# Transposes into PSUM, two row buffers, a new order in the MoE steps and 64x64 state products

## The reference

```python
# attention, one state of 64 x 64 per batch and head (4 x 8), 768 tokens each
state = gamma[None, :, None, None] * state + np.einsum('bhd,bhe->bhde', k[:, :, t], v[:, :, t])
y[:, :, t] = scale * np.einsum('bhd,bhde->bhe', q[:, :, t], state)
# MoE on x = y as 3072 tokens x 512, 8 experts, hidden width 1024
e_idx = np.argmax(x @ w_gate, axis=1)
out[mask] = gate_w[mask, None] * eom[mask, e, None] * (np.maximum(x[mask] @ w1[e], 0.0) @ w2[e])
# dense FFN, hidden width 2048
h = x @ w_in
return (h - np.tanh(h)) @ w_out
```

## Time and profile before

| | us |
|---|---|
| median of three runs | 1077.05 |
| lowest, highest | 1075.08, 1082.54 |
| profiled execution, its time | 1083.84 |
| its span, first to last instruction | 1082.1 |
| attention, MoE (from the span's start) | 0 to 145.4, 145.4 to 516 |
| PE, PEld, DVE, ACT, POOL busy in the span | 1037.4, 864.3, 722.2, 312.7, 390.9 |

### The profile page before, as it was taken

How to read it: one execution, slowest core, us unless ns; L and a number is a source line. 1 busy time by engine, 2 the same in 40 slices (tenths; PEclk the granted TensorE clock), 3 DMA queues, 4 the chain that set the end, 5 groups by cost and what they waited for, 6 DMA issues and landing times.

```text
span 1082.1 us, 18080 instructions
## 1 busy us (share of the span) xinstructions
PE 1037.4 (96%) x5424; PEld 864.3 (80%) x5425; DVE 722.2 (67%) x1247; ACT 312.7 (29%) x560; POOL 390.9 (36%) x325
## 2 busy tenths in 40 slices
PE   9999968989999999999789999999999999999998
PEld 8888857878888888787678887888887888888887
DVE  3666674654655556555478768877787886887775
ACT  2222212322323222231123333333334333333333
POOL 4377768585585995935700000000000000000000
PEclk9999988999999999999989999999999999999999
...
GB/s 332 278 315 307 254 152 223 223 240 213 242 234 223 273 262 221 259 204 165 81 10 11 20 39 19 19 0 48 19 10 48 16 13 39 19 0 0 40 1 39
DMA packets 70964, 138.28 MB, mean 128 GB/s; under 512 B 7056, under 2 KB 39184, under 8 KB 70928
## 3 DMA queue, kind: packets, MB, share of 16 engines
...
...
## 4 chain that ended last, share of the span: by engine, by line
PE 80%; DVE 8%; DMA 6%; issue 2%; ACTq 1%; ACT 1%; POOL 0%; DVEq 0%; SPq 0%; POOLq 0%
PE banks L1114 15%; PE banks L1116 15%; PE banks L1115 15%; PE banks L1206 8%; PE banks L1208 8%; PE banks L1207 8%; DMA hid_rows<-hid 2%; PE banks L1009 2%; PE banks L1053 2%; PE banks L1042 2%; DMA xs_sb<-x_sorted 2%; PE banks L1019 2%; PE banks L1027 2%; DVE xsT_lo L825 1%; DVE hidT L866 1%
## 5 line engine op out<-in xcount | busy, mean ns | idle before, releaser
L382 POOL TENSOR_TENSOR w_sb<-raw,w_sb 128x1024 fp32r<-128x1024 f32 x80 | 197.4, 2468 | 6.7
...
L1206 PE MATMUL banks<-x2T_hi,w_sb 128*128 (+1 forms) x384 | 153.0, 398 | 5.1 <-DVE g_sb L961 5.1
L1208 PE MATMUL banks<-x2T_lo,w_sb 128*128 (+1 forms) x384 | 150.7, 392 | 0.0
L1207 PE MATMUL banks<-x2T_hi,w_sb 128*128 (+1 forms) x384 | 150.5, 392 | 0.0
L1116 PE MATMUL banks<-w_sb,g_hi 128*128 128x512 f32 x384 | 149.4, 389 | 0.0
L1114 PE MATMUL banks<-w_sb,g_lo 128*128 128x512 f32 x384 | 149.4, 389 | 0.0
L1115 PE MATMUL banks<-w_sb,g_hi 128*128 128x512 f32 x384 | 149.4, 389 | 0.0
L1114 PE MATMUL banks<-w_sb,xsT_lo 128*128 (+1 forms) x248 | 100.8, 406 | 19.2 <-DVE xsT_lo L825 19.0
L633 ACT ACTIVATE square<-banks 128x512 f32<-128x512 f32 x96 | 57.4, 597 | 195.7 <-PE banks L1208 195.7
L640 ACT ACTIVATE g_hi<-g_sb 128x512 fp32r<-128x512 f32 x96 | 60.7, 632 | 164.5 <-PE banks L1116 146.8
L820 DVE STREAM_TRANSPOSE xsT<-xs_sb 128x512 f32<-128x512 f32 x31 | 22.0, 711 | 121.4 <-DMA xs_sb<-x_sorted 121.3
...
## 6 DMA issues: line engine op xcount, KB each, us to landing
...
```

The costliest lines, as they stand in the source:

```text
L382: nc.gpsimd.tensor_tensor(w_sb[:, s, 1, lo:hi], raw[:, p % RAW_SLOTS], w_sb[:, s, 0, lo:hi].bitcast(fp32), ALU.subtract).then_inc(piece_do ...
L1206: T.matmul(out_, w_lo, hi, start=first, stop=False)
L1207: T.matmul(out_, w_hi, hi, start=False, stop=False)
L1208: return T.matmul(out_, w_hi, lo, start=False, stop=last)
```

## The change

- **PSUM.** `xsT` and `hidT` move from SBUF to PSUM (bank 0, banks 3 and 6), so VectorE's transposes write PSUM and the splits read it. `xsT_hi` and `xsT_lo` get two sets each. Logits move from bank 4 to bank 7.
- **Order of a MoE step.** ScalarE does `x_hi(i+1)` first, VectorE the transpose of tile i+1 and `x_lo(i+1)` first.
- **Token scales.** VectorE's chain is cut into four groups, which stand behind its steps 0, 1, 2 and 3.
- **Attention.** `from_state` and `to_state` use one 64x64 block per head: eight products each in place of four. A chunk's output lies in banks 3 and 4, the order of the features in a row changes (`feature_order`, which the weights and tables follow), the state is copied by one activation, and the zeroing of `state_sb` goes. PE's loop over batches 1 and 2 is written out. In the last chunk `find_row` comes before the logits.

```diff
-    state_sb = b.place("state_sb", [P, 2, PAIRS, P])
+    state_sb = b.place("state_sb", [P, 2, PAIRS, HEAD_DIM])
...
-    xsT = c_.place("xsT", [P, DK, P])
-    xsT_hi = c_.place("xsT_hi", [P, DK, P], fp32r)
-    xsT_lo = c_.place("xsT_lo", [P, DK, P], fp32r)
+    xsT_hi = c_.place("xsT_hi", [P, 2, DK, P], fp32r)
+    xsT_lo = c_.place("xsT_lo", [P, 2, DK, P], fp32r)
...
-    hidT = c_.place("hidT", [P, FK, P])
...
-        logits = at(4)[:, 0:TOKEN_TILES * 2 * EXPERTS].rearrange("p (t e) -> p t e", t=TOKEN_TILES)
-        ranked = at(4)[:, TOKEN_TILES * 2 * EXPERTS:TOKEN_TILES * 2 * EXPERTS + 3 * EXPERTS].rearrange("p (n e) -> p n e", n=3)
+        logits_end = EXPERTS + TOKEN_TILES * 2 * EXPERTS
+        logits = at(7)[:, EXPERTS:logits_end].rearrange("p (t e) -> p t e", t=TOKEN_TILES)
+        ranked = at(7)[:, logits_end:logits_end + 3 * EXPERTS].rearrange("p (n e) -> p n e", n=3)
+        y_halves = at(3, 2).rearrange("p (h c) -> p h c", h=2)[:, :, 0:D // 2]
+        xsT = at(0)
+        hidT = [at(3), at(6)]
...
-                st = at(2).rearrange("p (a n) -> p a n", a=PAIRS)
-                for half in range(2):
-                    rows = slice(half * HEAD_DIM, (half + 1) * HEAD_DIM)
-                    nc.scalar.activation(state_sb[rows, c % 2, :, rows], st[rows, :, rows], ACT.Copy)\
-                      .then_inc(state_copied, 1)
+                nc.scalar.activation(state_sb[:, c % 2].rearrange("p a n -> p (a n)"), at(2)[:, 0:D // 2], ACT.Copy)\
+                  .then_inc(state_copied, 1)
...
-            act.wait_ge(state_zeroed, 1)
...
-            def x_hi(i):
+            def x_hi(i, number):
                 act.wait_ge(xsT_done, i + 1)
-                nc.scalar.activation(xsT_hi[:].rearrange("p a n -> p (a n)"), xsT[:].rearrange("p a n -> p (a n)"), ACT.Copy)\
+                if number >= 2:
+                    act.wait_ge(hid_done, i * 2 - 2)
+                nc.scalar.activation(xsT_hi[:, number % 2].rearrange("p a n -> p (a n)"), xsT, ACT.Copy)\
...
+                if number + 1 < MOE_TILES:
+                    x_hi(i + 1, number + 1)
                 relu(i, 0)
                 if number >= 3:
                     store_rows(i - 3)
                 relu(i, 1)
                 store_hidden(i, number)
-                if number + 1 < MOE_TILES:
-                    x_hi(i + 1)
...
+            moe_step(0, 0)
             act.wait_ge(shifted_done, 1)
             nc.scalar.activation(shifted[:], shifted[:], ACT.Exp).then_inc(exp_done, 1)
             nc.scalar.activation(per_tile[1][:], per_tile[0][:], ACT.Exp, scale=-1.0).then_inc(exp_done, 1)
-            for i in range(3):
+            for i in range(1, 3):
...
-            V.memset(state_sb[:], 0.0).then_inc(state_zeroed, 1)
...
-                V.tensor_tensor(xT_sb[:].rearrange("p a n -> p (a n)"), at(3), q_decay_sb[:, c], ALU.mult).then_inc(xT_made, 1)
+                V.tensor_tensor(xT_sb[:].rearrange("p (h a) n -> p h (a n)", h=2), y_halves,
+                                q_decay_sb[:, c].rearrange("p (h c) -> p h c", h=2), ALU.mult).then_inc(xT_made, 1)
...
+                    if last and c == CHUNKS - 1:
+                        find_row(t - 2)
                     if not first or c > 0:
                         add_logits(t - 1)
                         choose_expert(t - 1)
-                    if not first or c > 1:
+                    if (not first or c > 1) and not (last and c == CHUNKS - 1):
                         find_row(t - 2)
...
-            def x_lo(i):
+            def x_lo(i, par):
                 dve.wait_ge(xsT_hi_done, i + 1)
-                V.tensor_tensor(xsT_lo[:].rearrange("p a n -> p (a n)"), xsT[:].rearrange("p a n -> p (a n)"),
-                                xsT_hi[:].rearrange("p a n -> p (a n)").bitcast(fp32), ALU.subtract).then_inc(xsT_lo_done, 1)
+                V.tensor_tensor(xsT_lo[:, par].rearrange("p a n -> p (a n)"), xsT,
+                                xsT_hi[:, par].rearrange("p a n -> p (a n)").bitcast(fp32), ALU.subtract).then_inc(xsT_lo_done, 1)
...
+            def gate_scores():
+                link(V.tensor_tensor(gate_all[:], output_gate, onehot[:], ALU.mult))
...
+            def token_scales():
+                dve.wait_ge(exp_done, 2)
...
+            def rows_before():
+                first_tile, move = per_expert[0], per_expert[7]
...
+            def rows_after():
+                link(V.tensor_tensor(gate_all[:], last_start[:].unsqueeze(1).to_broadcast(over_tokens), onehot[:], ALU.mult))
...
-                    V.transpose(hidT[:, ks].rearrange("p k (b g) -> p g k b", g=QUADS),
+                    V.transpose(hidT[n].rearrange("p (k b g) -> p g k b", k=DK, g=QUADS),
                                 hid_quads[:].rearrange("p g (k a) -> p g k a", k=FK)[:, :, ks]).then_inc(hidT_done, 1)
...
             def moe_step(i, number):
+                if number + 1 < MOE_TILES:
+                    transpose_rows(i + 1)
+                    x_lo(i + 1, (number + 1) % 2)
                 if number >= 3:
                     if number >= 4:
                         dve.wait_ge(ys_stored, i * 16 - 48)
                     copy_rows(i - 3)
-                if number + 1 < MOE_TILES:
-                    transpose_rows(i + 1)
                 if number >= 1:
                     transpose_hidden(i - 1)
-                if number + 1 < MOE_TILES:
-                    x_lo(i + 1)
-                if number >= 1:
                     hid_lo(i - 1, (number - 1) % 2)
-            for i in range(5):
-                moe_step(i, i)
+            moe_step(0, 0)
+            gate_scores()
+            moe_step(1, 1)
+            token_scales()
+            moe_step(2, 2)
+            rows_before()
+            moe_step(3, 3)
+            rows_after()
+            moe_step(4, 4)
             with dve.Fori(5, MOE_TILES - 2, 2) as i:
                 moe_step(i, 5)
                 moe_step(i + 1, 6)
...
+            def head_place(pair, half):
+                group = (pair + half) % 2
+                return at(3 + half)[group * HEAD_DIM:(group + 1) * HEAD_DIM, pair // 2 * P:(pair // 2 + 1) * P]
+            def head_cols(pair, half):
+                return slice((2 * pair + half) * HEAD_DIM, (2 * pair + half + 1) * HEAD_DIM)
             def from_state(b, c):
-                pe.wait_ge(state_copied, b * (2 * (CHUNKS - 1)) + 2 * c)
+                pe.wait_ge(state_copied, b * (CHUNKS - 1) + c)
                 pe.wait_ge(xT_made, b * CHUNKS + c)
                 for pair in range(PAIRS):
-                    cols = slice(pair * P, (pair + 1) * P)
-                    T.matmul(at(3)[:, cols], state_sb[:, c % 2, pair], qT_sb[:, c % RING, cols],
-                             start=pair == 0, stop=False, skip_group_check=True)
+                    for half in range(2):
+                        rows = slice(half * HEAD_DIM, (half + 1) * HEAD_DIM)
+                        T.matmul(head_place(pair, half), state_sb[rows, c % 2, pair],
+                                 qT_sb[rows, c % RING, pair * P:(pair + 1) * P],
+                                 start=pair < 2, stop=False, skip_group_check=True)
             def to_state(b, c):
                 pe.wait_ge(kv_ready[c % RING], b * (16 * CHUNKS // RING) + 16 * (c // RING + 1))
                 pe.wait_ge(v_scaled_done, b * CHUNKS + (c + 1))
                 for pair in range(PAIRS):
-                    cols = slice(pair * P, (pair + 1) * P)
-                    last = T.matmul(at(2)[:, cols], kn_sb[:, c % RING, cols], v_scaled[:, c % RING, cols],
-                                    start=c == 0 and pair == 0, stop=True, skip_group_check=True)
+                    for half in range(2):
+                        cols = head_cols(pair, half)
+                        last = T.matmul(at(2)[half * HEAD_DIM:(half + 1) * HEAD_DIM, pair * HEAD_DIM:(pair + 1) * HEAD_DIM],
+                                        kn_sb[:, c % RING, cols], v_scaled[:, c % RING, cols],
+                                        start=c == 0 and pair == 0, stop=True, skip_group_check=True)
                 last.then_inc(kv_done, 1)
...
-                    for half in range(2):
-                        cols = slice((2 * pair + half) * HEAD_DIM, (2 * pair + half + 1) * HEAD_DIM)
-                        rows = slice(half * HEAD_DIM, (half + 1) * HEAD_DIM)
-                        last = T.matmul(at(3)[rows, pair * P:(pair + 1) * P], v_scaled[:, c % RING, cols],
-                                        probs[:, half * PAIRS + pair], start=c == 0 and pair == 0, stop=True,
+                    for half in (range(2) if pair % 2 == 0 else (1, 0)):
+                        last = T.matmul(head_place(pair, half), v_scaled[:, c % RING, head_cols(pair, half)],
+                                        probs[:, half * PAIRS + pair], start=c == 0 and pair < 2, stop=True,
                                         skip_group_check=True)
...
+                pe.wait_ge(onehot_done, t + 1)
```

(6 more changed lines are left out.)

82 lines of the change are left out of this document (41 added, 41 removed).

## The result

| us | before | after |
|---|---|---|
| median (lowest to highest), 4 runs each | 1079.6 (1075.08 to 1082.54) | 1163.84 (1156.45 to 1165.83) |
| profiled execution, its span | 1083.84, 1082.1 | 1162.94, 1161.2 |
| MoE from 145.4 us on | 370.6 | 450.6 |

The change makes the kernel slower by the ratio 1.0775 [1.0738, 1.0812]: 84 us by the medians, 79.1 us by the two profiled spans. 1150 was predicted.

What follows compares the result with a forecast made beforehand. TensorE was busy 94 to 95%; the new order was to put the row load's wait into ScalarE's MoE loop. +76.2 + 2.1 - 0.4 - 5.0 = +72.9 on 1077.05 gives 1150 us; range 1118 to 1182, 8 in 10: 1104 to 1182.

Steps and rivals of the forecast that it cites:

- The MoE step: MoE loop: a step grows from 11.31 to 14.24 us, +76.2 us over 26 steps.
- S to T: MoE: ScalarE's hidden-row store issue to VectorE's start transposing new rows; 10.17 us (10.37, less 0.7, plus 0.5).
- T to S: MoE: from VectorE's start of the row transpose to ScalarE's next hidden-row store issue; 4.07 us.
- the ring: MoE: store, reload, row load, transpose, x_hi, x_lo, copy, row store, relu follow in a loop; 14.24 us a step.
- Head and tail: MoE's ends: first steps +2.1 us, the 9.84 us token-scale hole filled and eaten within three steps; last step -0.4.
- Attention: State products in 64x64 blocks: gain capped by 0.32 us slack, 0.3 in 16 chunks, -5 us (bounds +5 and -5).
- PSUM at nothing: Transposes into PSUM priced at nothing in MoE, covered by VectorE's and ScalarE's idle time.
- The size of the wait: TensorE in MoE waits for VectorE's ys_sb copy ahead of rows_out, some 25 times about 3 us, 70 to 100 us.
- the rival on the clock: TensorE's clock halves in MoE gaps: 3.8 us spare absorbs 2.5; unrecovered 1320 us, partly recovered 1182 to 1220; chance 0.05.
- Quiet DMA: Rival, MoE: S to T falls to 7.63 to 8.7 us, step 11.7 to 12.8, total 1084 to 1113; chance 0.13.
- Faster: Rival, MoE: S to T under 6.8 us makes ScalarE's wait at x_hi free; total 1048 us; chance 0.05.
- The drains between shapes: Attention: tiling-mode changes drain TensorE; two drains of 0.1 us in 16 chunks would make -5 into -2.

Runs made afterwards that it cites:

- load_early: The changed kernel with ScalarE's load_rows(i+2) moved from the end of the step to right behind x_hi(i+1); 1068.03 us, 0.9913 of before.
- copy_first: The changed kernel with VectorE's copy_rows put back at the head of its step; 1117.82 us, 1.0368 of before.
- old_order: The changed kernel with ScalarE's and VectorE's MoE steps back in their old order, the rest of the change kept; 1064.45 us, 0.9871 of before.
- old_logits_first: old_order with VectorE's add_logits(t-1) moved ahead of mask_scores(t+1); 1054.21 us, 0.9769 of before.
- sbuf_old_order: old_order with xsT and hidT back in SBUF, the two sets of xsT_hi and xsT_lo kept; 1075.74 us, 0.9968 of before.

## Why the prediction came out as it did

**The MoE step: right, mechanism and size.** Predicted 14.24, measured 14.28. The halves erred against each other: S to T 10.17 predicted, 9.95 measured; T to S 4.07 against 4.33 (most steps 4.13 to 4.17, four of them 4.7 to 6.0). So the 0.04 between the two is in part luck, and no run shows the two corrections of S to T, -0.7 and +0.5, one by one. `load_early` and `copy_first` each take one piece out of the ring, and the step falls to TensorE's pace or by nearly that piece. `old_order` shows that the order accounts for all of the loss.

**Head and tail.** Head +2.1, measured 194.50 - 191.22 = +3.3. The hole of the earlier trace rows is filled and eaten, as said. Tail -0.4, measured 576.72 - 565.84 = 10.88, so about 0.

**The sum.** 26 x 2.97 = 77.2, and 3.3, is 80.5 against 79.1 of the spans. The medians differ by 84; the profiled execution of before lay above its median by 4, so the 5 us by which two spans and two medians disagree are spread of the runs.

**Attention: the step that failed**, by 5 us. I took the slack from the earlier trace rows as 0.32 us a chunk, from the end of L693 (61.87) to the start of `rows_and_logits` (62.24). TensorE does not start when the sums end but when it has heard: in after L692 ends at 62.65 and L1079 starts at 62.80, a hand-over of 0.15 and not 0.05. And behind the wait `rows_and_logits` itself takes 1.15 us (62.80 to 63.95) where it took 1.07 (62.24 to 63.31). The two take 0.18 off the 0.32 and leave 0.14. The better reading stood in the trace of before: its chunks with one product less last 5.08 against 5.22, which caps the gain at 0.14 in 16 chunks, 2.2 us. The products were not the mistake: half of 0.99 and 0.90 would be -0.95 (the prediction has -0.8), and they became about 0.67 shorter (0.60 and 0.62 in `old_logits_first`). And I did not ask what a faster TensorE runs into next at the start, where it is a table load.

**PSUM at nothing: right only in the new order.** With the old order, where TensorE sets the pace, it is worth 11 us. The prediction's cover, VectorE's idle time, was there on average, but x_lo stands directly ahead of a TensorE wait (14.1 us for `xsT_lo` in `sbuf_old_order`, 8.2 in `old_order`).

**The size of the wait.** Predicted 25 times about 3 us, 70 to 100; shown 20 times, 54.4 in all, or 69.5 with all that TensorE idles ahead of the `hidT_lo` products. TensorE filled part of the gap by running slower: some products behind a gap take 0.79 us at the low clock:

```profile
350.14 0.79 PE L1140 MATMUL banks<-w_sb,hidT_lo 128*128 x1 [5.67 <-DVE ys_sb L892]
```

That is the half clock of the earlier trace rows, at the mean 0.91 over the stage, in part of the steps. As the rival on the clock had it, the spare time takes this in, in all but a few steps: the ring passes through TensorE only in the four with a longer T to S, where a relu waits for it. In one of them, with S to T at 7.74:

```profile
318.82 0.60 ACT L580 ACTIVATE hid<-banks 128x512 f32<-128x512 f32 x1 [1.08 <-PE banks L1142]
```

The Trainium skill's "TensorE: Matmul & The Clock Gate" (Loop structure matters more than you think) names a long wait between the products of a loop as what lets the clock drop. The trace agrees as far as that slow products stand behind waits here, but no run ties a fall to a certain length of gap.

**The other rivals.** Quiet DMA: the shortest S to T is 7.67, but the mean hardly moved. Faster: the condition was S to T under 6.8, and `load_early` meets it (2.42) and is faster than before, but by 10 us and not 29: 1068 instead of 1048. The change did what it says.

**The drains between shapes.** Attention's result, near 0, can't tell -5 from -2, because the floor hides both. But `from_state` takes 0.60 us with a change of tile shape ahead of it and behind it, to `to_state` in after (61.12 to 61.72) as to `rows_and_logits` in `old_logits_first` (61.68 to 62.28), and at the rate of full-width records 16 of quarter the area would need 0.50. So around `from_state` both changes together cost some 0.1 us by this estimate. That isn't all: `rows_and_logits` behind the 64-wide products takes 1.18 us (62.28 to 63.46), where the same eight records took 1.07 behind full-width ones. The Trainium skill's "TensorEngine Tiling (Array Packing)", Key Properties, says that a change of tiling mode drains TensorE. These times don't contradict it: by them it would cost some 0.1 us a place at most, but no run isolates a drain.
